# Zero-padded rows of v, thresholds of two tiles at once on VectorE, and a new order of nine tiles in a fused attention kernel

## What is computed

```python
def _attn_ref(q, k, v, tau):
    scale = 1.0 / np.sqrt(q.shape[-1])
    scores = scale * np.matmul(q, k.transpose(0, 1, 3, 2))
    thresh = np.max(scores, axis=-1, keepdims=True) - tau
    scores = np.where(scores >= thresh, scores, -1000000000.0)
    scores = scores - np.max(scores, axis=-1, keepdims=True)
    attn = np.exp(scores)
    attn = attn / (np.sum(attn, axis=-1, keepdims=True) + 1e-09)
    return np.matmul(attn, v).astype(np.float32)
...
    x = np.ascontiguousarray(attn_out.transpose(0, 2, 1, 3)).reshape(B, S, H * D)
    x = _moe_ref(x=x, **moe_kwargs)
    return _moe2_ref(x=x, **moe2_kwargs)
```

## Time and profile before

| | |
|---|---|
| time, median of 3 runs | 1301.9 us (1301.14 to 1303.16) |
| time of the profiled execution | 1298.56 us |
| its span, first to last instruction | 1296.4 us |
| granted TensorE clock, mean | 0.999 of full |
| PE busy | 1274.4 us, 98% of the span |
| PEld busy | 1130.6 us, 87% |
| DVE, ACT, POOL busy | 895.6, 836.4 and 336.3 us |

### The profile page before, as it was taken

One profiled execution on the slowest core, in us unless ns is written; L12 is line 12 of the kernel. 1 busy time (PEld: TensorE's weight loads), 2 busy tenths in 40 slices (PEclk: granted clock), 3 DMA queues, 4 the chain that ended last, 5 costly groups with the idle time before them and its releaser, 6 DMA issues.

```text
span 1296.4 us, 29486 instructions
## 1 busy us (share of the span) xinstructions
PE 1274.4 (98%) x9396; PEld 1130.6 (87%) x9396; DVE 895.6 (69%) x1992; ACT 836.4 (65%) x2015; POOL 336.3 (26%) x371
## 2 busy tenths in 40 slices
PE   7999999999999999999999999999999999999998
PEld 7777877777777777779999999999999999999997
DVE  5777887877787877869576647666755756476644
ACT  5888888888888888865454444445435544454432
POOL 2566655566666554442000000000000000000000
PEclk9999999999999999999999999999999999999999
DMA  6566666666666676411101110110011011001000
GB/s 150 128 149 151 151 163 166 157 157 156 148 151 152 160 176 146 118 48 60 36 1 36 36 38 9 36 36 13 24 45 36 1 36 36 26 19 35 17 15 27
DMA packets 136828, 105.18 MB, mean 81 GB/s; under 512 B 91424, under 2 KB 108064, under 8 KB 136736
## 3 DMA queue, kind: packets, MB, share of 16 engines
q1 hardware_dynamic: 135232, 103.40, 31.0%
q10 hardware_dynamic: 1504, 0.62, 0.2%
HBM read 54.56 MB, written 19.02 MB: 57 GB/s over the span
## 4 chain that ended last, share of the span: by engine, by line
PE 94%; ACT 3%; DVE 1%; issue 1%; DMA 1%; SPq 0%; POOL 0%; ACTq 0%; DVEq 0%; POOLq 0%
PE score_ps L954 31%; PE score_ps L1040 16%; PE aux_ps L489 14%; PE aux_ps L572 13%; PE score_ps L530 12%; PE aux_ps L1024 8%; ACT k_raw L601 1%; PE aux_ps L499 1%; DMA q_all<-q_lo 1%; ACT probs L619 0%; PE score_ps L587 0%; DVE probs L690 0%; DVE neg_max L685 0%; DVE kk_lo L1168 0%; ACT threshold L617 0%
## 5 line engine op out<-in xcount | busy, mean ns | idle before, releaser
L685 DVE TENSOR_REDUCE neg_max<-score_ps 128x1 f32<-128x576 f32 x288 | 212.0, 754 | 71.8 <-PE score_ps L530 71.8
L690 DVE SCALAR_TENSOR_TENSOR probs<-score_ps,threshold,probs 128x576 f32<-128x576 f32 x288 | 228.0, 809 | 42.9 <-ACT probs L619 42.8
L530 PE MATMUL score_ps<-k_all,q_all 128*128 128x288 f32 x1280 | 232.8, 312 | 5.4 <-DVE probs L690 4.9
L954 PE MATMUL score_ps<-xm_hi,w_lo 128*128 128x288 f32 x768 | 226.1, 294 | 4.4 <-DVE x L1206 2.7
L954 PE MATMUL score_ps<-xm_hi,w_hi 128*128 128x288 f32 x768 | 226.6, 295 | 0.0
L954 PE MATMUL score_ps<-xm_lo,w_hi 128*128 128x288 f32 x768 | 226.4, 295 | 0.0
L619 ACT ACTIVATE probs<-score_ps,neg_max 128x576 f32<-128x576 f32 x288 | 212.5, 738 | 0.0
L530 PEld LDWEIGHTS score_ps<-k_all,q_all 128*128 128x128 f32 x1280 | 178.2, 189 | 11.3 <-DVE probs L690 6.3
L601 ACT ACTIVATE probsT<-aux_ps 128x512 f32<-128x512 f32 x288 | 164.3, 597 | 34.9 <-PE aux_ps L489 30.7
L489 PE MATMUL aux_ps<-ident,probs 128*128 128x128 f32 x1280 | 185.4, 276 | 0.7 <-ACT probsT_rem L601 0.6
L489 PEld LDWEIGHTS aux_ps<-ident,probs 128*128 128x128 f32 x1280 | 148.3, 141 | 19.4 <-ACT probsT L601 15.2
(11 more groups left out here) (88 smaller groups left out, 2377.1 us busy)
## 6 DMA issues: line engine op xcount, KB each, us to landing
k_all<-k_all SPq DMA_DIRECT2D x31, 320.0 KB, 4.4
q_all<-q_lo SPq DMA_DIRECT2D x62, 160.0 KB, 3.7
recip_rows<-recip_scratch SPq DMA_DIRECT2D x64, 144.0 KB, 4.4
x_scratch<-x_out SPq DMA_DIRECT2D x32, 288.0 KB, 2.1
out<-y SPq DMA_DIRECT2D x36, 256.0 KB, 2.0
k_all<-k_all SPq DMA_DIRECT2D x31, 288.0 KB, 3.5
v_nat<-in_v SPq DMA_DIRECT2D x32, 256.0 KB, 3.6
qk_nat<-in_q SPq DMA_DIRECT2D x63, 128.0 KB, 2.6
```

The costliest lines, as they stand in the source:

```text
L530: last = nc.tensor.matmul(ps[:, half, 0:HALF], query(h, i, par), kk[par][:, at:at + HALF], start=(n == 0), stop=(n == len(terms) - 1))
L685: nc.vector.tensor_reduce(neg_max[:, i:i + 1], scored(i), mybir.AxisListType.XY, ALU.max, negate=True).then_inc(max_ready, 1)
L690: nc.vector.scalar_tensor_tensor(tile_halves(i), scored(i), threshold[:, i:i + 1], tile_halves(i), ALU.is_ge, ALU.mult, accum_out=row_sum[ ...
L954: last = nc.tensor.matmul(ps, w, m, start=(n == 0), stop=(n == 3 * len(terms) - 1))
```

## The change

Four things are changed in the attention, none in the mixing layers.

1. **v.** `v_nat` loses its ninth block, and a new buffer `v_rem` has a block for each head, zeroed once by POOL. The last 64 rows of a head's v are loaded into their half of the partitions, and the other half stays zero. The last step of each `pv` now takes all 128 rows of `probsT_rem` and `v_rem`. PE's first instruction, and SP's first load of v, wait for the zeroing.
2. **Thresholds.** The nine small instructions on ACT are gone. DVE makes thresholds for two tiles at once, in the order of its maxima (`thr0` to `thr4`, five a pair, the last for one tile).
3. **Order.** The tiles are now taken as 3 1 2 4 0 8 6 7 5 on all engines, and `k`, `kq`, `q`, `probs`, `rem` and `pv` stand at new places in the three lists and in the drain lists.
4. **Slots.** A tile's slot in PSUM is now its turn modulo 3, not its number modulo 3. The program for SP is otherwise the same, in the same order.

```diff
--- before.py
+++ after.py
...
 PE_PLAN = steps("""
-    probs5- scores1 k0 kq0 scores0 pv0- q0 scores2 probs6- scores4 rem1- probs4- scores3 probs7-
-    probs8- scores5 probs2 pv1- probs1 scores7 probs0 rem0 scores6 scores8 probs3
+    scores3 kq0 probs2- scores1 k0 pv0- probs4- scores2 q0 scores4 rem1- probs5- scores0 probs1
+    scores8 probs7- probs6- scores6 probs8- probs3 scores7 pv1- probs0 scores5 rem0
 """)
 ACT_PLAN = steps("""
-    probs3- probs5- k0 exp8- kq0 exp1 exp0 pv0- q0 probs6- exp2 rem1- probs4- probs7- probs8- exp4
-    exp5 exp3 probs2 pv1- probs1 probs0 exp7 rem0 exp6
+    rem0- kq0 probs2- exp5- exp1 k0 exp3 pv0- probs4- q0 exp2 rem1- probs5- exp4 probs1 exp0 probs7-
+    probs6- probs8- exp6 probs3 exp8 exp7 pv1- probs0
 """)
 DVE_PLAN = steps("""
-    max8- max1 max0 mask8- sum0- recip0- mask1 max2 mask0 max4 mask2 max3 max5 mask5 mask4 mask3 max7
-    max6 mask7 mask6
+    mask7- max5- thr4- max3 max1 mask5- sum0- thr0 recip0- mask1 mask3 max2 max4 thr1 mask2 max0
+    mask4 max8 thr2 mask0 max6 max7 mask8 thr3 mask6
 """)
...
 SCORE_TURN = ranked(PE_PLAN, "scores")
+BY_TURN = sorted(SCORE_TURN, key=SCORE_TURN.get)
 MAX_TURN = ranked(DVE_PLAN, "max")
 EXP_TURN = ranked(ACT_PLAN, "exp")
+THRESHOLDS = [range(n, min(n + 2, TILES)) for n in range(0, TILES, 2)]
 MASK_TURN = ranked(DVE_PLAN, "mask")
...
-        v_nat = sb("v_nat", [P, 2, TILES, D])
+        v_nat = sb("v_nat", [P, 2, MIX, D])
+        v_rem = sb("v_rem", [P, 2, 2, D])
         probsT = sb("probsT", [P, FULL, 2, S])
...
         def scored(i):
-            return score_ps[i % SLOTS][:, :, 0:HALF]
+            return score_ps[SCORE_TURN[i] % SLOTS][:, :, 0:HALF]
         def count(it, c, per_pair, local):
...
         def load_head(eng, n, name, it, c, h, loaded):
...
         def load_v(eng, it, c):
-            load(eng, v_nat[:, c % 2, :, :], "v", it, c, v_loaded[c % 2])
+            par = c % 2
+            eng.dma_start(v_nat[:, par, :, :].rearrange("p (h t) d -> p h (t d)", h=2),
+                          heads["v"][bass.ds(it * 4 + 2 * c, 2), 0:MAIN, :].rearrange(
+                              "h (p t) d -> p h (t d)", t=FULL)).then_inc(v_loaded[par], 16)
+            for h in range(2):
+                eng.dma_start(v_rem[REM * h:REM * (h + 1), par, h, :],
+                              heads["v"][it * 4 + (2 * c + h), MAIN:S, :]).then_inc(v_loaded[par], 16)
         def stack_q(eng, it, c):
...
+            sp.wait_ge(ident_made, 3)
             load_v(sp, 0, 0)
...
             nc.gpsimd.memset(q_all[1][:, QW:H1].bitcast(F32), 0.0).then_inc(ident_made, 1)
-            pool.wait_ge(ident_made, 2)
+            nc.gpsimd.memset(v_rem[:], 0.0).then_inc(ident_made, 1)
+            pool.wait_ge(ident_made, 3)
             nc.gpsimd.affine_select(out=ident[:], in_=ident[:], compare_op=ALU.not_equal, fill=1.0,
...
         def tensor(pe):
-            pe.wait_ge(ident_made, 3)
+            pe.wait_ge(ident_made, 4)
             def transpose(out, in_):
...
-                        if i >= SLOTS:
-                            pe.wait_ge(probs_ready, count(it, cc, TILES, MASK_TURN[i - SLOTS] + 1))
+                        turn = SCORE_TURN[i]
+                        if turn >= SLOTS:
+                            pe.wait_ge(probs_ready, count(it, cc, TILES, MASK_TURN[BY_TURN[turn - SLOTS]] + 1))
                         elif cc > 0:
-                            pe.wait_ge(probs_ready, count(it, cc - 1, TILES, MASK_TURN[i - SLOTS + TILES] + 1))
-                        ps = score_ps[i % SLOTS]
+                            pe.wait_ge(probs_ready, count(it, cc - 1, TILES, MASK_TURN[BY_TURN[turn - SLOTS]] + 1))
+                        ps = score_ps[turn % SLOTS]
                         parts = (i % 2,) if i < MIX else (0, 1)
...
                             for h in range(2):
-                                rows = slice(0, P) if t < FULL else slice(REM * h, REM * (h + 1))
-                                m = probsT[:, t, h, cols] if t < FULL else probsT_rem[rows, cols]
+                                m = probsT[:, t, h, cols] if t < FULL else probsT_rem[:, cols]
+                                values = v_nat[:, cc % 2, h * FULL + t, :] if t < FULL else v_rem[:, cc % 2, h, :]
                                 last = nc.tensor.matmul(bank[D * h:D * (h + 1), 0:cols.stop - cols.start],
-                                                        v_nat[rows, cc % 2, h * FULL + t if t < FULL else MIX, :],
-                                                        m, start=(t == 0), stop=(t == FULL))
+                                                        values, m, start=(t == 0), stop=(t == FULL))
                     elif kind == "hidden":
-                        pe.wait_ge(probs_ready, count(it, PAIRS - 1, TILES, MASK_TURN[6 + i // 2] + 1))
+                        pe.wait_ge(probs_ready, count(it, PAIRS - 1, TILES, MASK_TURN[BY_TURN[6 + i // 2]] + 1))
                         pe.wait_ge(w_split, 2 * UNITS + 2)
...
                     if kind == "exp":
                         act.wait_ge(max_ready, count(it, cc, TILES, MAX_TURN[i] + 1))
-                        nc.scalar.activation(threshold[:, i:i + 1], neg_max[:, i:i + 1], ACT.Identity,
-                                             bias=tau_down[:, 0:1], scale=-1.0).then_inc(threshold_ready, 1)
+                        turn = MAX_TURN[i]
                         nc.scalar.activation(tile_halves(i), scored(i), ACT.Exp,
-                                             bias=neg_max[:, i:i + 1], scale=1.0).then_inc(exp_done, 1)
+                                             bias=neg_max[:, turn:turn + 1], scale=1.0).then_inc(exp_done, 1)
                     elif kind == "probs":
...
             run(FIRST_PREPARE, 0, 0)
-            act.wait_ge(tau_steps, 2)
             walk(run, act, ACT_PLAN, ACT_DRAIN, ACT_EXTRA)
         def vector(dve):
...
                     if kind == "max":
                         dve.wait_ge(scores_full, count(it, cc, TILES, SCORE_TURN[i] + 1))
-                        nc.vector.tensor_reduce(neg_max[:, i:i + 1], scored(i), mybir.AxisListType.XY, ALU.max,
+                        turn = MAX_TURN[i]
+                        nc.vector.tensor_reduce(neg_max[:, turn:turn + 1], scored(i), mybir.AxisListType.XY, ALU.max,
                                                 negate=True).then_inc(max_ready, 1)
+                    elif kind == "thr":
+                        turns_of = THRESHOLDS[i]
+                        group = slice(turns_of.start, turns_of.stop)
+                        dve.wait_ge(max_ready, count(it, cc, TILES, turns_of.stop))
+                        nc.vector.tensor_scalar(threshold[:, group], neg_max[:, group], -1.0, tau_down[:, 0:1],
+                                                ALU.mult, ALU.add).then_inc(threshold_ready, 1)
                     elif kind == "mask":
-                        dve.wait_ge(threshold_ready, count(it, cc, TILES, EXP_TURN[i] + 1))
+                        turn = MAX_TURN[i]
+                        dve.wait_ge(threshold_ready, count(it, cc, len(THRESHOLDS), turn // 2 + 1))
                         dve.wait_ge(exp_done, count(it, cc, TILES, EXP_TURN[i] + 1))
                         nc.vector.scalar_tensor_tensor(
-                            tile_halves(i), scored(i), threshold[:, i:i + 1], tile_halves(i),
+                            tile_halves(i), scored(i), threshold[:, turn:turn + 1], tile_halves(i),
                             ALU.is_ge, ALU.mult,
...
                     elif kind == "mix":
...
                                             ALU.subtract).then_inc(q_steps, 1)
+            dve.wait_ge(tau_steps, 2)
             walk(run, dve, DVE_PLAN, DVE_DRAIN, DVE_EXTRA)
         return Engines(sync, gpsimd, tensor, scalar, vector)
```

More of the change, by code:

```diff
@@ L238, in prepared @@
             return 1 + max(number(run, x) for x in FIRST_PREPARE)
-        def load(eng, nat, name, it, c, loaded):
-            eng.dma_start(nat[:, 0:2 * FULL, :].rearrange("p (h t) d -> p h (t d)", h=2),
-                         heads[name][bass.ds(it * 4 + 2 * c, 2), 0:MAIN, :].rearrange(
-                             "h (p t) d -> p h (t d)", t=FULL)).then_inc(loaded, 16)
-            for h in range(2):
-                eng.dma_start(nat[REM * h:REM * (h + 1), MIX, :],
-                             heads[name][it * 4 + (2 * c + h), MAIN:S, :]).then_inc(loaded, 16)
         def load_head(eng, n, name, it, c, h, loaded):
```

13 lines of the change are left out of this document (8 added, 5 removed).

## The result

The changed kernel takes 1314.4 us (median of 4 runs, 1313.71 to 1315.24) against 1301.6 us before: a ratio of 1.0098, with a 95% interval of 1.0082 to 1.0114. The prediction was 1306.5 us, with a range up to 1312. The sign was right, and the size was not: +12.8 us in place of +4.8.

What follows compares the result with a forecast made beforehand. The prediction took a loop through SP's queue, ending in the queries' landing, as the bound. 30 x 0.14 + 0.3 + 0.3 = +4.8 us on 1301.9 us, rounded to 1306.5 us, range 1299 to 1312.

Steps and rivals of the forecast that it cites:

- The bound: At turn 0 of each pair, the queries' landing, set by SP's order, releases PE's scores; 17.21 us a pair.
- wait at turn 0: PE's wait for the queries' landing before turn-0 scores, read as 0.15 us a pair.
- PE part of the loop: PE's work from turn-0 scores to the transpose of the reciprocals: 6.97 us, forecast to grow by 0.14 us a pair.
- the loop: Turn-0 scores, PE's work to the reciprocals' transpose, ACT's copy, SP, queries' landing, next turn-0 scores: 17.21 us.
- padding: Zero-padded v saves one switch, 0.15 us for each `pv`; only `pv0-` stands inside the loop.
- order: Four groups of four transposes inside the loop instead of three: +0.44 us a pair, less the `pv0-` wait that goes.
- wait of `pv0-`: PE's wait at `pv0-` for the copy of the keys, 0.12 to 0.20 us a pair, which goes in the new order.
- SP part: From the reciprocals' transpose through ACT's copy and SP to the next turn-0 scores: stays 10.24 us, bounds 10.1 and 10.5.
- Thresholds: Nine instructions off ACT, five onto DVE at 0.27 us each, neither on the loop: 0 to +0.3 us a pair.
- Ends: Pair 1's first turn-0 tile later by 0.3 us, and +0.3 us after the last turn-0 tile.
- A: Rival: PE's work, not the loop, is the bound; 1283 to 1293 us, best 1289, chance 0.15.
- C: Rival: ACT's copy of the reciprocals comes late by 0.1 to 0.4 us in each pair; 1310 to 1318 us, chance 0.13.

Runs made afterwards that it cites:

- e9: The kernel before (old order) with zero-padded v and thresholds of two tiles at once on VectorE as tensor_reduce: 1293.8 us, ratio 0.9934.
- e3_threshold_as_reduce: The changed kernel with its five threshold instructions a pair as tensor_reduce in place of tensor_scalar, same places and waits: 1303.95 us, ratio 1.0017.

## Why the prediction was off, step by step

**The bound: right, by a thin margin.** SP's order set the queries' time, PE's 94% notwithstanding: exchanging two steps on SP gained 4.4 us. But of the 0.15 us a pair that the prediction read as a wait at turn 0 the period gave back 0.07, as PE alone needs 17.19 us a pair in the old order. Here PE's busy share of 99% came nearer to the truth (17.19 of 17.26 us) than the 77% of the weight loads.

**PE part of the loop: right.** Forecast +0.14 us on 6.97 in the new order. It is 7.12 in the changed kernel and 7.10 with the reduction. Its two terms hold one by one, in means over the pairs, which alternate by 0.09 us before: padding -0.15 (forecast -0.15), order +0.26, from 6.84 in the old order with padding and reduction (e9) to 7.10 (forecast 0.44 less 0.12 to 0.20, which is 0.24 to 0.32). The wait of `pv0-` was misread by a little: 0.82 against 0.63 + 0.09 leaves 0.10 us, not 0.12 to 0.20.

**SP part: nearly.** Forecast unchanged at 10.24 us, measured 10.14 with the reduction. ACT, rid of nine instructions, copies the reciprocals 0.08 us sooner. The prediction priced that relief at nothing ("Neither is on the loop"), but the copy of the reciprocals is on it. It cancels most of the +0.14: the period is 17.26 us without the hold.

**Thresholds: the step that failed.** "Neither is on the loop: cost nothing, from 0 to +0.3 us a pair". Two errors are in it. The price came from a mean over one operation in one place, 0.271 us, and `thr1` costs 0.98. And the bound looked only for a mask that is late before the reciprocals (`scores4`). The late one stands behind them (`scores8`), in the half that I had taken to be covered by SP's loop. A cover has a size: 0.50 us here, and the stall is 0.88. In numbers the term is +10.4 us, more than the 7.9 us that were missed (without the hold the time is 1303.95 us, 2.5 under the forecast), and the end of its bound (0.3 x 30 = 9 us) was left out of the range.

The trace of before showed the hold, and in the very row that gave the price. The addition to the row sums takes 0.17 us where POOL is idle, but 30 of its 32 rows in the kernel before take longer, up to 0.286 us, and end 0.02 to 0.03 us behind a cast of POOL. Its group over all the pairs, then one row of DVE and the row of POOL over it:

```profile
L698 DVE TENSOR_SCALAR row_sum<-row_sum x32: 173/275/286, 33.8 to 568.3; 128x9 f32<-128x9 f32 x32
```

```profile
223.71 0.28 DVE L698 TENSOR_SCALAR row_sum<-row_sum 128x9 f32<-128x9 f32 x1
```

```profile
223.24 0.72 POOL L426 CAST k_all<-k_raw 128x640 fp32r<-128x640 f32 x1 [3.11 <-ACT q_raw L605]
```

How long such a hold can get, another row tells. Behind the last pair DVE squares tiles; one of them met POOL's multiplication. DVE, then POOL, of the kernel before:

```profile
580.75 1.56 DVE L1164 TENSOR_TENSOR square<-relu 128x288 f32<-128x288 f32 x1
...
582.73 0.44 DVE L1164 TENSOR_TENSOR square<-relu 128x288 f32<-128x288 f32 x1
```

```profile
580.43 1.57 POOL L445 TENSOR_TENSOR x_out<-x_raw,recip_rows 128x512 f32<-128x512 f32 x1 [5.64 <-DMA recip_rows<-recip_scratch]
```

The same instruction takes 0.44 and 1.56 us. It is of another form than the thresholds, a `tensor_tensor`, and ends 0.3 us behind POOL's. A look at single rows and at what POOL does over them, not at a mean, would have given the bound: up to the rest of a POOL instruction of 1.5 us.

**Ends: mis-sized.** Forecast +0.3 and +0.3 us. The first copy of the reciprocals is at 37.5 to 39.1 us in five profiles of the old order with thresholds on ACT, and at 39.3 to 40.9 in six of the new order, +1.6 in the mean; the last pair and what follows it take 1.7 us more. The order is not all of the +1.6: three profiles of the old order with thresholds on VectorE have the first copy at 39.0 to 40.3 us, and the granted clock of the head differs from profile to profile. At the head, the first tile that needs a freed slot (turn 3) starts at 18.70 us before and at 20.30 after. In the new order its slot is freed by the second mask, `mask3`, as `mask1` goes first. PE of before, and of after:

```profile
18.70 0.80 PE L530 MATMUL score_ps<-k_all,q_all 128*128 128x288 f32 x4 [1.70 <-DVE probs L690]
```

```profile
20.30 1.31 PE L539 MATMUL score_ps<-k_all,q_all 128*128 128x288 f32 x8 [2.98 <-DVE probs L704]
```

That the order of the two masks is the cause was not tried.

**Rivals.** A (PE's own work bounds) is what comes once SP and the hold are out of the way: 1287.55 us, inside its 1283 to 1293. C gave the right time, 1310 to 1318, for the wrong reason: ACT is not late for the reciprocals in the changed kernel (0.31 us), and is so with the thresholds back on ACT (0.48). The terms as measured: padding -5.9, thresholds without the hold -2.4, order +10.2 with its ends (5.4 us of it in the loop, 29 x (17.26 - 17.08)), hold +10.4, together +12.3 us of 12.8.

## What to carry to other kernels

A small VectorE operation costs what it waits for. Before one is added beside a busy GpSimd, look for the longest row of its kind in the trace, and for rows that end just behind one of GpSimd's, and choose a form that is not held; here the same result as a `tensor_reduce` saved 10 us. "Beside the loop" is a cover with a size: work out its margin in microseconds, and set every new stall against it. And where a queue that only issues DMAs closes a loop, the cheapest gain is to issue first what the next round waits for: with that and an unheld threshold the changed kernel runs in 1287.55 us, 1.0% less than before.

## What the runs showed of the hardware that was not expected

- A VectorE `tensor_scalar` on 128x2 values took 0.22 us alone and up to 1.7 us beside GpSimd, and each of the 135 that took over 0.3 us ended within 0.03 us behind a GpSimd instruction; a `tensor_reduce` that gives the same numbers took 0.147 to 0.158 us in all 160 cases of e3_threshold_as_reduce, 62 of them wholly inside a GpSimd instruction.
- Cutting two GpSimd subtractions of 1.47 us in four each made 3.79 us out of 2.94, about 0.14 us for each further instruction.
- On TensorE, a step of 128 rows in place of 64 at the end of a `pv` saved 0.15 us each (2.46 to 2.31 us and 2.99 to 2.84 us for a whole `pv`), of which the loop through SP let at most one of two through (5.9 us a kernel, and 8.3 us without that loop).
